# Linear attention, soft mixture of experts and FFN in one kernel: expert weights placed anew, slot denominators moved ahead, the FFN's first tile by quarters

## The chip, the core and the metric

The kernel runs on one core of a Trainium2 chip. Five engines work in parallel, each on its own instruction queue: TensorE (PE, matrix products; its weight loads are shown as PEld), VectorE (DVE), ScalarE (ACT), GpSimd (Pool) and SyncE (SP), which in this kernel issues all DMAs. They are tied together by semaphores only: an instruction waits until a counter has reached a value. PE writes its results to PSUM, eight banks of 128 x 512 fp32; DVE and ACT carry them to SBUF. The metric is the time of one execution on the device in microseconds; lower is better. It is given as the median of several runs.

## What is computed

Three stages, cut to the core:

```python
def attn(r, k, v, w, u):            # B, H, S, D = 4, 8, 768, 48
    for t in range(S):
        kv = einsum('bhd,bhe->bhde', k[t], v[t])
        y[t] = einsum('bhd,bhde->bhe', r[t], state + u * kv)
        state = w * state + kv

def moe(x, phi, w1, w2):            # x: 3072 x 384, 8 experts with 4 slots each, F = 1024
    logits = x @ phi                              # 3072 x 32
    d = exp(logits - logits.max(0)); d /= d.sum(0)      # over the tokens
    slot_in = d.T @ x                             # 32 x 384
    slot_out[e] = relu(slot_in[e] @ w1[e]) @ w2[e]
    c = exp(logits - logits.max(1)); c /= c.sum(1)      # over the slots
    return c @ slot_out

def ffn(x, w_in, w_out):            # 384 -> 2048 -> 384
    h = x @ w_in
    return where(h > 0, h, exp(min(h, 0)) - 1) @ w_out
```

## The kernel before

**Attention** runs over 24 units: 6 chunks of 128 tokens times 4 batches (`un = c * B + b`). For each unit SP loads r, k and v (192 KB each), Pool multiplies them by decay tables (L435 to L453), PE turns them and forms scores, outputs and states, and DVE and ACT carry results along. SP issues everything in one order, written out in `load_chunk`: with every unit also one piece of the first expert weight, `load_w1(un)` (L329, 24 pieces of 512 KB in all). A load of r and k for unit un + 4 waits for `bonus_ready` and `k_scaled`, a load of v for `y_done`.

**Expert stage.** After the last unit DVE forms the softmax over the tokens (`col_w`) and over the slots (`row_w`), PE sums the slots' inputs (L618, `x_sb` weighted by `col_w`, with one column of ones for the denominators), and DVE turns the sums into `slot_T` through `den_cols`, `slot_parts` and `den_inv`. `row_parts` holds `row_w` split in a rounded part and a rest, each twice; PE turns it to `c_T`. The experts work in two groups of four: `expert_in(g, n)` (L635), a ReLU on ACT and DVE, `expert_turn` and `expert_out` (L654), which waits at its first four products for `w2_loaded[e]`. The order on PE is in(0), in(1), out(0), first half of out(1), turn of group 0's result, second half of out(1), turn of group 1's. The second expert weights (`w2_sb`, 8 of 1536 KB, L366) are loaded into places that other tensors leave: 0 and 1 where r and k were, 2 to 4 over `x_sb` after the slot sums (`PE_SLOT_IN`), 5 to 7 over w1 after `h_done` 1 and 2. Behind them in SP's queue come `w_in` (3 of 1 MB, L384) and, after `so_done` 1, `w_out` (4 of 768 KB, L388).

**FFN.** Since x @ w_in is c @ (slot_out @ w_in), the kernel forms G = slot_out @ w_in (L704, a 32 x 2048 matrix, kept as four row groups of bank 3, one for each 512 columns), splits it into a rounded part and a rest (`G_parts`) and spreads each group over 128 rows by two matmuls with 0/1 matrices (`spread`, L718), so that `G_T` (128 x 2048) meets `c_T` in one product. `ffn_in(i, f)` (L712) then gives tile f (128 of the 2048 columns of h) of chunk i (512 tokens). Each tile passes exp (ACT L1109), relu(1 - exp) (ACT L1096), max(h, 0) minus that (DVE L973), rounding to `elu_hi` (DVE L986) and the rest `elu_lo` (DVE L965), and enters the output by 12 matmuls (L753 to L755): for each of four batches hi x w_out_hi, hi x w_out_lo, lo x w_out_hi. There are 96 tiles, 16 for each of 6 chunks. `w_out_high(f)` on ACT (L1084) rounds w_out's rows, and Pool forms the rest `w_out_lo` (L461), in the first chunk only. All orders are written out by hand; `RING = 4` banks hold h.

## Time and profile before

| | |
|---|---|
| runs | 411.21 us median of 3 (410.6 to 412.23) |
| profiled execution | 413.13 us, of which the span (first to last instruction) is 410.8 |
| granted TensorE clock, mean | 0.992 |
| PE busy | 388.4 us (95%) |
| DVE busy | 275.1 us (67%) |
| ACT busy | 221.2 us (54%) |
| Pool busy | 117.5 us (29%) |
| read from HBM | 45.86 MB |

The page of the profile gives each engine's busy time and, in 40 slices of the span (10.3 us each), its busy share in tenths, the clock that TensorE was granted (9 is 90% or more of full speed) and the share of the 16 DMA engines that was busy. Roughly: attention until 132 us, the softmaxes and experts until 175, G and the first tiles until 195, the FFN loop to the end. The trace gives every instruction with its start, its duration and what it waited for.

### The profile page before, as it was taken

To read this page: it belongs to the slowest core of one execution; us is meant where nothing else is said; L and a number is where in the kernel's file an instruction comes from. 1 tells how busy PE (TensorE), PEld (TensorE's weight loads), DVE (VectorE), ACT (ScalarE), POOL (GpSimd) and SP (SyncE) were. 2 spreads that over 40 slices of the span, in tenths; PEclk is the share of its full clock that TensorE was granted. 3 is DMA by queue.
4 is the path that set the end of the run, shared out by engine and by line. 5 is a ranking of instruction groups with operands and counts; after the bars stand their busy time and mean duration, and the time that the engine had idled before them with its cause. 6 is when DMAs were issued, how large, how long until landed. Compare 5 with 4: busy or idle time off the path is not lost.

```text
span 410.8 us, 9542 instructions
## 1 busy us (share of the span) xinstructions
PE 388.4 (95%) x3529; PEld 343.2 (84%) x3529; DVE 275.1 (67%) x517; ACT 221.2 (54%) x503; POOL 117.5 (29%) x131
## 2 busy tenths in 40 slices
PE   6699999999998798769999999999999999999997
PEld 6588888888885344238999999999999999999996
DVE  4687777777764920049997677676767767676771
ACT  1676767676763216057665545645554564546441
POOL 4997878787850000018530000000000000000000
PEclk9899999999999999899999999999999999999999
DMA  6999999999977499950002000200020020002002
GB/s 126 204 234 228 245 234 239 237 225 243 218 231 300 145 429 356 406 201 2 0 2 77 2 1 2 77 0 0 0 77 0 0 77 0 0 0 77 2 0 77
DMA packets 86530, 51.05 MB, mean 124 GB/s; under 512 B 76768, under 2 KB 82016, under 8 KB 85088
## 3 DMA queue, kind: packets, MB, share of 16 engines
q1 hardware_dynamic: 86496, 50.59, 42.9%
q8 instruction: 23, 0.38, 0.4%
q14 instruction: 11, 0.09, 0.1%
HBM read 45.86 MB, written 4.72 MB: 123 GB/s over the span
## 4 chain that ended last, share of the span: by engine, by line
PE 88%; DVE 4%; DMA 3%; POOL 1%; issue 1%; ACT 1%; SPq 0%; POOLq 0%; DVEq 0%
PE psum L753 16%; PE psum L754 16%; PE psum L755 16%; PE psum L504 6%; PE psum L535 6%; PE psum L712 5%; PE psum L543 3%; DMA w<-in_moe_w_dram 3%; PE psum L516 3%; PE psum L486 3%; PE psum L635 3%; PE psum L493 3%; PE psum L526 2%; PE psum L654 2%; PE psum L550 1%
## 5 line engine op out<-in xcount | busy, mean ns | idle before, releaser
L753 PE MATMUL psum<-w_out_hi,elu_hi 128*128 128x384 f32 x384 | 129.3, 337 | 1.1 <-DVE elu_lo L965 1.1
L754 PE MATMUL psum<-w_out_lo,elu_hi 128*128 128x384 f32 x384 | 129.0, 336 | 0.0
L755 PE MATMUL psum<-w_out_hi,elu_lo 128*128 128x384 f32 x384 | 128.3, 334 | 0.0
L1109 ACT ACTIVATE exp_h<-psum 128x512 f32<-128x512 f32 x96 | 57.6, 601 | 98.3 <-PE psum L712 98.3
L973 DVE SCALAR_TENSOR_TENSOR elu<-psum,neg_part 128x512 f32<-128x512 f32 x96 | 66.2, 690 | 54.5 <-ACT neg_part L1096 54.4
L753 PEld LDWEIGHTS psum<-w_out_hi,elu_hi 128*128 128x128 f32 x384 | 72.1, 188 | 3.7 <-DVE elu_lo L965 2.5
L754 PEld LDWEIGHTS psum<-w_out_lo,elu_hi 128*128 128x128 f32 x384 | 72.0, 188 | 3.3
L755 PEld LDWEIGHTS psum<-w_out_hi,elu_lo 128*128 128x128 f32 x384 | 72.1, 188 | 0.0
L965 DVE TENSOR_TENSOR elu_lo<-elu,elu_hi 128x512 fp32r<-128x512 f32 x96 | 66.3, 691 | 0.1
L1096 ACT ACTIVATE neg_part<-exp_h 128x512 f32<-128x512 f32 x96 | 59.9, 625 | 0.0
L1004 ACT ACTIVATE scores<-ident,bonus 128x128 f32<-128x128 f32 x192 | 58.7, 390 | 0.8 <-DVE bonus L804 0.7
L986 DVE CAST elu_hi<-elu 128x512 fp32r<-128x512 f32 x96 | 49.7, 517 | 0.1
L814 DVE COPY_PREDICATED scores<-mask,psum 128x512 f32<-128x512 uint32 x48 | 35.4, 740 | 14.1 <-ACT scores L1004 13.6
L461 POOL TENSOR_TENSOR w_out_lo<-w_out_raw,w_out_hi 128x384 fp32r<-128x384 f32 x16 | 20.2, 1277 | 73.5 <-ACT w_out_hi L1084 73.5
L712 PE MATMUL psum<-c_T,G_T 128*128 (+1 forms) x96 | 37.4, 393 | 1.0 <-DVE elu L973 1.0
L504 PE MATMUL psum<-r_pair,k_pair 64*128 64x128 f32 x384 | 28.8, 290 | 1.8 <-DVE k_pair L809 0.9
L504 PEld LDWEIGHTS psum<-r_pair,k_pair 64*128 64x128 f32 x384 | 24.3, 193 | 3.9 <-issue 1.8
L453 POOL TENSOR_TENSOR k_nat<-k_raw,k_table 128x384 f32<-128x384 f32 x23 | 23.1, 1004 | 12.2 <-PE psum L526 12.2
L535 PE MATMUL psum<-scores,v_sb 128*64 128x128 f32 x384 | 26.3, 279 | 0.0
L440 POOL TENSOR_TENSOR r_raw<-r_raw,u_row 128x384 f32<-128x384 f32 x24 | 24.5, 1019 | 6.1 <-DVE r_nat L796 4.3
L1009 ACT COPY y_T<-psum 128x512 f32<-128x512 f32 x24 | 14.1, 586 | 22.2 <-PE psum L535 22.2
L442 POOL TENSOR_TENSOR r_raw<-r_raw,k_raw 128x384 f32<-128x384 f32 x24 | 24.0, 1001 | 1.9
(126 smaller groups left out, 409.0 us busy)
## 6 DMA issues: line engine op xcount, KB each, us to landing
w_sb<-in_moe_w_dram SPq DMA_DIRECT2D x24, 512.0 KB, 4.9
w<-in_moe_w_dram SPq DMA_DIRECT2D x8, 1536.0 KB, 9.8
r_raw<-in_r_dram SPq DMA_DIRECT2D x24, 192.0 KB, 4.6
k_raw<-in_k_dram SPq DMA_DIRECT2D x24, 192.0 KB, 5.1
v_sb<-in_v_dram SPq DMA_DIRECT2D x24, 192.0 KB, 5.3
out_dram<-out_sb SPq DMA_DIRECT2D x24, 192.0 KB, 1.9
w_in_sb<-in_moe_w_in_dram SPq DMA_DIRECT2D x3, 1024.0 KB, 16.0
w_out_raw<-in_moe_w_out_dram SPq DMA_DIRECT2D x4, 768.0 KB, 14.2
```

Of the source, the lines that this page charges most:

```text
L504: m = pe.matmul(ps_A[two][:, a, :], k_pair[rows, i, a, :], r_pair[rows, i, a, :], start=True, stop=True)
L535: m = pe.matmul(ps_y[e0:e0 + HP, two, (a // 2) * P:(a // 2) * P + P], v_sb[:, b, h, :], scores[:, i, h, :], start=(first and a < 2), stop= ...
L712: pe.matmul(banks[4 + f % RING][:, :], G_T[:, f * P:(f + 1) * P], c_T[:, bass.ds(i * BANK, BANK)], start=True, stop=True).then_inc(ffn_don ...
L753: pe.matmul(acc, hi, w_out_hi[:, f, :], start=(f == 0), stop=False)
L754: pe.matmul(acc, hi, w_out_lo[:, f, :], start=False, stop=False)
L755: m = pe.matmul(acc, lo, w_out_hi[:, f, :], start=False, stop=(f == KF2 - 1))
L965: dve.tensor_tensor(elu_lo[:, f % RING, :], elu[:, f % 2, :], elu_hi[:, f % RING, :].bitcast(F32), ALU.subtract).then_inc(lo_done, 1)
L973: dve.scalar_tensor_tensor(out=elu[:, f % 2, :], in0=banks[4 + f % RING][:, :], scalar=0.0, in1=neg_part[:, f % 2, :], op0=ALU.max, op1=AL ...
L986: dve.tensor_copy(elu_hi[:, f % RING, :], elu[:, f % 2, :]).then_inc(hi_done, 1)
L1004: m = act.activation(scores[:, i, h, :], ident[:, :], ACT.Copy, scale=bonus[:, i, h:h + 1])
L1096: act.activation(neg_part[:, f % 2, :], exp_h[:, f % 2, :], ACT.Relu, bias=1.0, scale=-1.0).then_inc(neg_ready, 1)
L1109: act.activation(exp_h[:, f % 2, :], banks[4 + f % RING][:, :], ACT.Exp).then_inc(exp_done, 1)
```

## The change

Five things, none of which changes the arithmetic of a result except the order in which w1's rows are added.

1. w1 is loaded in 8 pieces of 1536 KB, one for each expert, at units 1, 4, ..., 22, instead of 24 of 512 KB. Partition p holds the rows 3p to 3p+2 of an expert, so the slots' inputs are turned with a stride of three columns.
2. The second weights get other places. Weight 2 lies behind weights 0 and 1 and is loaded when the last unit's y is done; weights 3 and 4 lie over the first two thirds of `x_sb` and are loaded when PE has read 8 and 16 of its 24 units (`x_used`); 5 and 6 after `h_done` 1, 7 after `h_done` 2. `row_parts` moves behind 3 and 4, `w_out_lo` to the place of 5 and 6.
3. On DVE the slot denominators and `slot_T` come ahead of the sums of the rows.
4. G's split is on DVE alone, first 128 columns, then 384. Only the first 512 columns are spread by PE, with 32 rows instead of 128. The other 1536 columns of `G_T` are copied from `G_parts` by twelve DMAs of 32 x 512 (64 KB) on SP's queue; PE waits for them (`G_moved`) before tiles 4, 8 and 12 of the first chunk.
5. The first tile passes by quarters of 128 tokens, with its own semaphores: product, exp, relu, max-subtract, rounding, rest, and its three matmuls for each batch as soon as that quarter is there. In tiles 1 and 2 of the first chunk PE takes the eight products of `elu_hi` before the four of `elu_lo`.

```diff
         cursor[0] = max(cursor[0], LATE_AT)
+        w2_sb += [place("w2_2", [P, KF1, DM], F32)]
...
-        w2_sb += [place(f"w2_{e}", [P, KF1, DM], F32) for e in range(2, 5)]
+        w2_sb += [place(f"w2_{e}", [P, KF1, DM], F32) for e in range(3, 5)]
+        assert cursor[0] <= X_AT + 2 * UNITS // 3 * XW * 4
+        row_parts = place("row_parts", [P, UNITS, 4, SLOTS], F32R)
...
-        w1_dram = w1.rearrange("e (c p) f -> p (e c) f", p=P)
+        w1_dram = w1.rearrange("e (p c) f -> e p c f", p=P)
...
                     un = c * B + b
-                    load_w1(un)
+                    if un % KD == 1:
+                        load_w1(un // KD)
...
-            sp.wait_ge(pe_step, PE_SLOT_IN)
-            for e in range(2, 5):
-                load_w2(e)
+            sp.wait_ge(y_done, UNITS)
+            load_w2(2)
+            sp.wait_ge(x_used, 1)
+            load_w2(3)
+            sp.wait_ge(x_used, 2)
+            load_w2(4)
             sp.wait_ge(h_done, 1)
             load_w2(5)
+            load_w2(6)
             sp.wait_ge(h_done, 2)
-            for e in range(6, E):
-                load_w2(e)
+            load_w2(7)
...
+            sp.wait_ge(G_parts_ready, 4)
+            for n in range(1, F2 // BANK):
+                for j in range(GROUPS):
+                    sp.dma_start(G_T[j * GW:(j + 1) * GW, n * BANK:(n + 1) * BANK].bitcast(F32),
+                                 G_parts[n * GW:(n + 1) * GW, j % 2, :].bitcast(F32)).then_inc(G_moved[n], 16)
...
+                if n in (1, 3):
+                    m.then_inc(x_used, 1)
...
-            spread_G(0)
-            spread_G(1)
-            spread_G(2)
+            spread_G(banks[0][:, 0:P], slice(0, P))
             pe.wait_ge(cT_ready, UNITS // 4)
             pe.wait_ge(G_first_ready, 1)
-            ffn_in(0, 0)
-            spread_G(3)
-            for f in range(1, RING):
-                ffn_in(0, f)
-            pe.wait_ge(G_ready, F2 // BANK - 1)
+            ffn_in_first(0)
+            ffn_in_first(1)
+            pe.wait_ge(G_parts_ready, 4)
+            spread_G(banks[1][:, 0:BANK - P], slice(P, BANK))
+            ffn_in_first(2)
+            ffn_in_first(3)
...
+            pe.wait_ge(w_out_ready, 1)
+            first_out_high(0)
+            pe.wait_ge(G_rest_ready, 1)
+            for b in range(1, B):
+                pe.wait_ge(elu_first, b + 1)
+                ffn_in(0, b)
+                first_out_high(b)
+                first_out_low(b - 1)
+            first_out_low(B - 1).then_inc(parts_used, 1)
...
-            act.wait_ge(G_done, 1)
-            act.copy(G_parts[:, 0, :], banks[3][:, :]).then_inc(G_parts_ready, 1)
             w_out_high(0)
+            w_out_high(1)
             act.wait_ge(G_spread, 1)
-            act.copy(G_T[:, 0:BANK], banks[0][:, :]).then_inc(G_first_ready, 1)
+            act.copy(G_T[:, 0:P], banks[0][:, 0:P]).then_inc(G_first_ready, 1)
+            for b in range(B):
+                quarter = slice(b * P, (b + 1) * P)
+                act.wait_ge(h_first, b + 1)
+                act.activation(exp_h[:, 0, quarter], banks[4 + b][:, 0:P], ACT.Exp).then_inc(exp_first, 1)
+                act.wait_ge(exp_first, b + 1)
+                act.activation(neg_part[:, 0, quarter], exp_h[:, 0, quarter], ACT.Relu, bias=1.0, scale=-1.0
+                               ).then_inc(neg_first, 1)
```

In SP's queue behind attention, before (w2_n is expert weight n; the number behind the last underscore counts buffers):

```order
L366 DMA w2_1_81<-in_moe_w2_dram 128x3072
L366 DMA w2_2_97<-in_moe_w2_dram 128x3072 [waits pe_step]
L366 DMA w2_3_98<-in_moe_w2_dram 128x3072
L366 DMA w2_4_99<-in_moe_w2_dram 128x3072
L366 DMA w2_5_101<-in_moe_w2_dram 128x3072 [waits h_done]
L366 DMA w2_6_106<-in_moe_w2_dram 128x3072 [waits h_done]
L366 DMA w2_7_107<-in_moe_w2_dram 128x3072
```

and in SP's queue of the changed kernel, to the end of the loads:

```order
L382 DMA w2_1_81<-in_moe_w2_dram 128x3072
L382 DMA w2_2_82<-in_moe_w2_dram 128x3072 [waits y_done]
L382 DMA w2_3_97<-in_moe_w2_dram 128x3072 [waits x_used]
L382 DMA w2_4_98<-in_moe_w2_dram 128x3072 [waits x_used]
L382 DMA w2_5_101<-in_moe_w2_dram 128x3072 [waits h_done]
L382 DMA w2_6_102<-in_moe_w2_dram 128x3072
L382 DMA w2_7_105<-in_moe_w2_dram 128x3072 [waits h_done]
L403 DMA w_in_sb_108<-in_moe2_w_in_dram 128x2048 x3
L407 DMA w_out_raw_109<-in_moe2_w_out_dram 128x4x384 [waits so_done]
L407 DMA w_out_raw_109<-in_moe2_w_out_dram 128x4x384 x3
L413 DMA G_T_104<-G_parts_106 32x512 [waits G_parts_ready]
L413 DMA G_T_104<-G_parts_106 32x512 x11
```

Weights 2 to 4 wait for three earlier events instead of one, weight 6 goes with 5, and twelve copies of G stand behind w_out.

On DVE after the clearing of `slot_T`, before:

```order
L905 TENSOR_REDUCE row_sum<-row_w 128x24 [waits act_step]
L907 TENSOR_SCALAR row_sum<-row_sum 128x24 [waits dve_step]
L909 RECIPROCAL row_sum<-row_sum 128x24 [waits dve_step]
L911 TENSOR_TENSOR row_w<-row_w,row_sum 128x768 [waits dve_step]
L915 COPY den_cols<-psum 128x128 [waits pe_step]
L916 COPY slot_parts<-psum 128x384
L918 TENSOR_SCALAR den_inv<-psum 128x32 [waits pe_step]
L921 RECIPROCAL den_inv<-den_inv 128x32 [waits dve_step]
L924 TENSOR_TENSOR slot_T<-psum,den_inv 128x24x4 [waits pe_step,dve_step]
L930 CAST row_hi<-row_w 128x768 [waits dve_step]
```

and on DVE in the changed kernel:

```order
L975 COPY den_cols<-psum 128x128 [waits pe_step]
L976 COPY slot_parts<-psum 128x384
L978 TENSOR_SCALAR den_inv<-psum 128x32 [waits pe_step]
L981 RECIPROCAL den_inv<-den_inv 128x32 [waits dve_step]
L984 TENSOR_TENSOR slot_T<-psum,den_inv 128x24x4 [waits pe_step,dve_step]
L990 TENSOR_REDUCE row_sum<-row_w 128x24 [waits act_step]
L992 TENSOR_SCALAR row_sum<-row_sum 128x24 [waits dve_step]
L994 RECIPROCAL row_sum<-row_sum 128x24 [waits dve_step]
L996 TENSOR_TENSOR row_w<-row_w,row_sum 128x768 [waits dve_step]
L999 CAST row_hi<-row_w 128x768 [waits dve_step]
```

The four row steps have moved behind `slot_T`, on which PE waits.

On PE after G's sum, before:

```order
L718 MATMUL psum<-G_parts,spread 128x512 [waits G_parts_ready,spread_ready]
L718 MATMUL psum<-G_parts,spread 128x512 x5
L712 MATMUL psum<-c_T,G_T 128x512 [waits G_first_ready,cT_ready]
L718 MATMUL psum<-G_parts,spread 128x512 x2
L712 MATMUL psum<-c_T,G_T 128x512 x3
L712 MATMUL psum<-c_T,G_T 128x512 [waits elu_done,G_ready]
L753 MATMUL psum<-w_out_hi,elu_hi 128x384 [waits w_out_ready,lo_done]
```

and on PE in the changed kernel:

```order
L751 MATMUL psum<-G_parts,spread 128x128
L745 MATMUL psum<-c_T,G_T 128x128 [waits G_first_ready,cT_ready]
L745 MATMUL psum<-c_T,G_T 128x128
L751 MATMUL psum<-G_parts,spread 128x384 [waits G_parts_ready]
L751 MATMUL psum<-G_parts,spread 128x384
L745 MATMUL psum<-c_T,G_T 128x128 x2
L770 MATMUL psum<-w_out_hi,elu_hi 128x384 [waits hi_first,w_out_ready]
L770 MATMUL psum<-w_out_lo,elu_hi 128x384
L740 MATMUL psum<-c_T,G_T 128x512 [waits elu_first,G_rest_ready]
L770 MATMUL psum<-w_out_hi,elu_hi 128x384 [waits hi_first]
...
L775 MATMUL psum<-w_out_hi,elu_lo 128x384 [waits lo_first] x2
L740 MATMUL psum<-c_T,G_T 128x512 [waits G_moved1]
```

The first output matmul stands behind 128-column steps only, and ffn_in(0, 4) waits for copied pieces of G.

## Rows read from the trace of the kernel before

**Rows 1.** Page, the span in 40 slices: granted clock and DMA share, in tenths

```profile
PEclk9899999999999999899999999999999999999999
DMA  6999999999977499950002000200020020002002
```

**Rows 2.** Timeline and tile view, attention: start us, us, engine, line; us to landing

```profile
92.66 0.38 SPq L322 DMA_DIRECT2D r_raw<-in_r_dram  x1
...
DMA to landing us min/median/max: 3.1/4.6/5.0
...
101.03 1.02 POOL L435 TENSOR_TENSOR r_nat<-r_raw,r_table 128x384 f32<-128x384 f32 x1
```

**Rows 3.** Timeline, 134 to 145 us: PE, DVE, ACT

```profile
134.60 4.10 PE L618 MATMUL psum<-x_sb,col_w 128*32 128x386 f32 x48 [1.44 <-ACT col_w L1044]
...
137.12 0.95 DVE L905 TENSOR_REDUCE row_sum<-row_w 128x24 f32<-128x768 f32 x1
...
139.54 0.28 DVE L915 COPY den_cols<-psum 128x128 f32<-128x128 f32 x1
...
140.32 0.30 ACT L1049 CAST ident_r<-ident 128x128 fp32r<-128x128 f32 x1 [3.23 <-PE psum L623]
...
142.94 1.75 DVE L934 TENSOR_TENSOR row_parts<-row_w,row_hi 128x1536 fp32r<-128x1536 f32 x1
```

**Rows 4.** Timeline of expert_out on PE; then windows (busy, clock, DMA share, GB/s)

```profile
156.67 6.39 PE L654 MATMUL psum<-w,hidden_T 128*32 128x384 f32 x70
...
165.94 4.30 PE L654 MATMUL psum<-w,hidden_T 128*32 128x384 f32 x26 [2.89 <-DMA w<-in_moe_w_dram]
...
170.76 2.79 PE L654 MATMUL psum<-w,hidden_T 128*32 128x384 f32 x32
...
168.00:169.00 1.00, 1.00 (x9) 0.36 (x2) 0.00 (x0) 0.00 (x0) 0.00 (x0) 0.50 1.01 426
```

**Rows 5.** DMA issues on SP, w2 and w_out: first and last start; us to landing

```profile
w<-in_moe_w_dram SPq DMA_DIRECT2D x1, 1536.0 KB, 6.1
...
L366 SPq DMA_DIRECT2D w<-in_moe_w_dram x2: 432/432/432, 139.1 to 139.6; - x2
...
DMA to landing us min/median/max: 9.5/11.8/14.2
...
L366 SPq DMA_DIRECT2D w<-in_moe_w_dram x1: 328/328/328, 147.1 to 147.1; - x1
...
DMA to landing us min/median/max: 10.2/10.2/10.2
...
L366 SPq DMA_DIRECT2D w<-in_moe_w_dram x2: 327/380/433, 153.5 to 153.9; - x2
...
DMA to landing us min/median/max: 8.7/10.3/12.0
...
L388 SPq DMA_DIRECT2D w_out_raw<-in_moe_w_out_dram x4: 378/1373/6626, 162.1 to 169.7; - x4
...
w_out_raw<-in_moe_w_out_dram SPq DMA_DIRECT2D x1, 768.0 KB, 11.9
```

**Rows 6.** Timeline and chain, 177 to 196 us; last, phi's issues (us to landing)

```profile
177.91 0.59 ACT L1087 CAST G_parts<-psum 128x512 fp32r<-128x512 f32 x1 [3.81 <-PE psum L704]
...
184.57 0.44 PE L753 MATMUL psum<-w_out_hi,elu_hi 128*128 128x384 f32 x1 [0.62 <-DVE elu_lo L965]
...
187.61 0.44 PE L753 MATMUL psum<-w_out_hi,elu_hi 128*128 128x384 f32 x1 [0.45 <-DVE elu_lo L965]
...
190.06 1.23 DVE L986 CAST elu_hi<-elu 128x512 fp32r<-128x512 f32 x1
...
185.99 7.59 POOL L461 TENSOR_TENSOR w_out_lo<-w_out_raw,w_out_hi 128x384 fp32r<-128x384 f32 x6 [0.41 <-ACT w_out_hi L1084]
...
195.38 0.18 PE psum L753
...
phi_sb<-in_moe_phi_dram SPq DMA_DIRECT2D x4, 12.0 KB, 2.3
```

More of the change, by code:

```diff
@@ new lines, in _, with first_out_high, first_out_low @@
+            ffn_in_first(2)
+            ffn_in_first(3)
+            def first_out_high(b):
+                pe.wait_ge(hi_first, b + 1)
+                for n, w_part in enumerate((w_out_hi, w_out_lo)):
+                    pe.matmul(banks[b][:, 0:DM], elu_hi[:, 0, b * P:(b + 1) * P], w_part[:, 0, :],
+                              start=(n == 0), stop=False)
+            def first_out_low(b):
+                pe.wait_ge(lo_first, b + 1)
+                return pe.matmul(banks[b][:, 0:DM], elu_lo[:, 0, b * P:(b + 1) * P], w_out_hi[:, 0, :],
+                                 start=False, stop=False)
@@ L743, in ffn_group @@
                         ffn_in(i + 1, f + RING - KF2)
-                    pe.wait_ge(lo_done, q + 1)
+                    if first and f == 0:
+                        continue
+                    if first and f <= 2:
+                        pe.wait_ge(hi_done, q)
+                        pe.wait_ge(w_out_ready, f + 1)
+                        for b in range(B):
+                            for w_part in (w_out_hi, w_out_lo):
+                                pe.matmul(banks[b][:, 0:DM], elu_hi[:, f % RING, b * P:(b + 1) * P], w_part[:, f, :],
+                                          start=False, stop=False)
+                        pe.wait_ge(lo_done, q)
+                        for b in range(B):
+                            m = pe.matmul(banks[b][:, 0:DM], elu_lo[:, f % RING, b * P:(b + 1) * P], w_out_hi[:, f, :],
+                                          start=False, stop=False)
+                        m.then_inc(parts_used, 1)
+                        continue
+                    pe.wait_ge(lo_done, q)
                     if first:
@@ new lines, in first_lo @@
+            def first_lo(b):
+                dve.wait_ge(hi_first, b + 1)
+                return dve.tensor_tensor(elu_lo[:, 0, quarter(b)], elu[:, 0, quarter(b)],
+                                         elu_hi[:, 0, quarter(b)].bitcast(F32), ALU.subtract).then_inc(lo_first, 1)
+            first_elu(0)
+            first_hi(0)
+            dve.wait_ge(G_spread, 2)
+            dve.tensor_copy(G_T[:, P:BANK], banks[1][:, 0:BANK - P]).then_inc(G_rest_ready, 1)
+            for b in range(1, B):
+                first_elu(b)
+                first_lo(b - 1)
+                first_hi(b)
@@ L975, in ffn_group @@
                                              ).then_inc(elu_done, 1)
[L976 removed]
+                    if not (first and f <= 2):
                         elu_lo_of(i, (f - 1) % KF2, q - 1)
[L978 removed]
+                    dve.wait_ge(elu_done, q)
                     if f >= RING:
```

150 lines of the change are left out of this document (90 added, 60 removed).

## Prediction, written before the changed kernel ran

> **What bounds the kernel now.** I read the slices first [rows 1]: TensorE's granted clock is at the upper level (2.4 GHz) nearly everywhere, with one dip in the seventeenth slice, and the DMA share is at its ceiling up to about 123 us and again from 139 to 180 us, with a hole between. Then the chain of waits: it is TensorE for 88% of the span, but between 138 and 188 us it passes through VectorE's softmax rows, through one DMA of 12.0 us (expert weight 7), and through the hand-overs ACT to DVE to ACT at the head of the FFN. From 195.4 us on it is TensorE alone. So every microsecond by which that point comes earlier is a microsecond of the kernel, and nothing after it matters. The FFN loop itself is not changed. I therefore work out when expert weight 7 is there, when G is there, and when the fifth FFN tile (f = 4) starts.
>
> **Attention stage.** The 24 pieces of w1 (512 KB) become 8 (1536 KB) at units 1, 4, ..., 22. The bytes are the same; what has been issued ahead of a load of r differs by one old piece at most, early or late, which at 430 GB/s is 1.2 us. The load of r for unit 20 is issued at 92.66 and lands 4.6 us later (median, 5.0 at most), and Pool first reads it at 101.03 [rows 2]: 3.4 to 3.8 us to spare, and no engine in this stage waits for a DMA. Cost: nothing, hidden by those 3.4 us. Without that cover it costs what a load comes late, eight times; that is the rival on the slow side. Below zero it could bring little, since nothing there waits for a transfer; I allow 0.3.
>
> **Slot denominators first.** VectorE does row_sum (0.95, with two short steps after it) and the row_w product before den_cols; PE's slot sums (L618) are ready at 138.7, but den_cols starts at 139.54 [rows 3]. Moved behind slot_T, the row steps free the path: gain 139.54 - 138.72 = **0.8**. The row steps take 2.5 us, so row_parts ends near 142.94 + 1.75 + 2.5 - 0.8 - 0.2 = 146.2 instead of 144.7. Who waits for that: the ReLU of `hidden` on the same queue, which can't start before expert_in(0) is done at 147.1 - 0.8 = 146.3, and the weights' turn on PE at 153. Both hide it. Were the cover gone it would be 0.1 or so.
>
> **Expert weights.** Group 1's first half is 32 records of L654, and the second half shows what 32 cost: 2.79 us. Group 0 ends at 162.0, so the half should end at 164.7; its last 26 records start at 165.94 and take 4.30, until 170.25 [rows 4]. Lost: **5.5** us. 26 records at 2.79/32 are 2.27, so 2.0 of the 5.5 is the clock: PE was idle from about 163 to 165.9 and the granted clock was 0.50 (1.2 GHz) in 168 to 169 [rows 4]. The other 3.5 is the wait.
> Does weight 7 come in time now? Landings before [rows 5]: weight 2 issued 138.75 into an empty queue, 6.1 later; 3 and 4 at 148.6 and 153.8; 5 at 157.3; 6 at 162.2; 7 at 165.9. In a full queue they are 3.5 to 5.2 apart, mean 4.1. After: weight 2 is issued behind 1 as soon as the last unit's y is done, some 6 us ahead of the rest; weight 3 at the first x_used (8 of the 24 units of L618 [rows 3], 134.6 + 4.1 x 8/24 = 136.0), weight 4 at 137.4. They fill the hole and land by about 146.3. 5 and 6 go at expert_in(0)'s end, 146.3, into a queue just empty: 152.4 and 156.5. 7 follows at 160.6 (159.4 to 162.6 by the two ends of the interval). PE first wants it 0.2 us into group 1, which is now 162.0 - 0.8 + 0.2 = 161.4. So the wait becomes 0 to 1.2; I take 0.2, nearest to the mean interval. What is late next is w_in: 1 MB each, 2/3 of 4.1 apart, the last at 168.8, wanted at 170; it hides. Gain 5.5 - 0.2 = **5.3**. G's sum then ends at 177.9 - 0.8 - 5.3 = 171.8.
>
> The Trainium skill, "DMA: Bandwidth & Descriptors" (Latency and other measured facts), says that two of the sixteen DMA engines are usually slower in traces. The landings agree so far as they can: the mean rate shows weights 2 to 5 moved by 155.5, while weight 5 is only reported at 157.3. By the mean rate alone weight 7 would be there near 158 and the 0.2 would be 0.
>
> **Head of the FFN, with T = end of G's sum.** Before, T = 177.9: G_parts starts at T+0.0 and the first output matmul at T+6.7 [rows 6]. After, the same steps are 128 columns wide: 0.30 on ACT, 0.28 on VectorE from PSUM [rows 3], about 0.3 for one matmul. In a row: two on VectorE (T+0.65), spread with PE's start (T+1.2), G_T on ACT (1.6), product (2.0), exp and relu (2.65), max-subtract and rounding (3.2): first output matmul at **T+3.35**. That is not the gain. VectorE then has one 384-wide copy and ten 128-wide steps in a row, about 0.27 each: until T+6.5. Only then comes tile 1, full width, and there VectorE is already the limit before: PE starts tile 1 at 187.61, right behind elu_lo, and the period is 2.58 because the rounding step takes 1.23 instead of 0.43 while Pool runs w_out_lo [rows 6]. Pool is just as busy after. I lay it out: tile 1's rounding ends T+7.65 and its low part T+8.35; tile 2's T+10.1 and 11.3; tile 3's low part, 2.6 on, T+14.1. PE: tile 0 done T+7.0 (before T+8.9), tile 1 T+9.85, tile 2 T+12.3, then it waits for tile 3's low part until T+14.15, and starts tile 4 at T+16.5 to 16.7. Before that was 195.38, T+17.5. Gain 17.5 - 16.6 = **0.9**. Ends: 0, if the many narrow steps cost 0.1 more each; and 1.9, the lead at the end of tile 0 kept whole.
>
> The Trainium skill, "SBUF — State Buffer" (Who interferes with whom), says that VectorE's copies in a two-port mode, and its operations with two inputs in SBUF, exclude GpSimd for the whole instruction. The 1.23 agrees. By that rule the narrow steps of tile 0 run free, since ACT makes w_out_hi(2) only after them; it gives the same sum.
>
> **G by DMA.** Three wide VectorE copies (1.93 in all) and six of eight spread matmuls go; twelve DMAs of 64 KB come, behind G_parts_ready 4 at T+1.9 on SP's queue. Behind them on SP are only the stores, 40 us later. PE waits for the first four before ffn_in(0, 4), wanted at T+7.0, harmful from T+7.25 = 179.0. No such transfer is in the trace; bounds: the four small phi loads take 2.3 us to land [rows 6], and w_out's four pieces are in the same queues ahead. Those landed last at 169.7 + 11.9 = 181.6 [rows 5], 15.7 behind weight 7, with the queue full all the way; after, 160.6 + 15.7 = 176.3. So the four pieces land between T+1.9 + 4 x 0.4 + 2.3 = 177.6 and, if they start only behind w_out, 176.3 + 2.3 = 178.6. Cost 0, with 0.4 to 1.4 us of cover; that is the thinnest cover of the change. w_out's first piece (landed 175.5 before) comes at 170.2, ahead of T, and its two roundings on ACT are off the path.
>
> By the skill's "DMA: Bandwidth & Descriptors" (Anatomy of one DMA) a DMA costs a fixed 2.0 us or so plus its bytes; four pieces by that page are an estimate of 2.6 us, at 177.9.
>
> **Sum.** 0.8 + 5.3 + 0.9 = 7.0. The profiled execution took 413.13 with a span of 410.8; it becomes 406.1. The median of the runs is 411.21, 1.9 below the profiled one, so the forecast is 411.21 - 7.0 = **404.2**.
>
> **Rivals.** (a) Forecast as above, 403.1 to 405.4: chance 0.56. (b) Expert weight 7 is late still: w2 intervals of 5 us and a slower start out of the empty queue, 1.5 to 4 us of wait, with 2.0 for the clock if PE is idle 3 us again. For it: intervals of 4.9 and 5.2 exist. Against: three weights leave 9 to 2 us earlier. Typical 404.2 + 2.5 = 406.7, at worst 410.2: 0.15. (c) G's pieces wait behind w_out, or cost more than the phi loads: 1 to 3 us of PE waiting at tile 1, 406.2: 0.13. (d) The clock falls in the sparse stretch T to T+4, where PE has some 1.5 us of work; before, with 3 to 4 us in the first 6, it stayed at 1.00. At half clock tiles 0 and 1 cost 2 more: 406.2: 0.03. (e) The head gains its full lead, since PE works on high parts while VectorE catches up: 411.21 - 0.8 - 5.5 - 1.9 = 403.0: 0.08. (f) Slower: bursts of w1 in attention. A burst puts 1 MB more ahead of r (2.4 us), and if a queue that is full cannot make this up in the two units without one, loads land over 3.6 us late. From 3.6 + 9.1/8 = 4.7 us late on, eight bursts eat the 7.0 and 2.1 more and the kernel is over 0.5% slower; at 5.0 us late they cost 11.2, 415.4: 0.03. (g) The change doesn't do what it says, no wait goes because slots 5 to 7 still follow h_done: gains 0.8 + 0.9, 409.5: 0.02.
>
> **Numbers.** The range 401.9 to 407.3 takes (a), (c), (d), (e) and most of (b), and 0.8 for the scatter of the runs shown. About 0.5% (2.1 us) is what a measurement of this kernel tells from no change: faster than 409.15 are (a), (c), (d), (e) and nearly all of (b): 0.92. Within: the rest of (b), (g), and half-way cases of (f): 0.05. Slower: 0.03.
>
> **What would show it.** den_cols starts at 138.7; the wait of L654 for DMA under 1 us and PEclk without its dip; G's first rounding near 172; the first output matmul 3.3 us later; the first full-width rounding on VectorE at T+7; PE's wait before ffn_in(0, 4) at zero; the fifth tile at T+16.6. Wrong would make it: Pool waiting for r or k in attention, a dip of the clock past T, or PE waiting on G_T's DMAs.

## Result and the profile after

| | before | changed |
|---|---|---|
| median of 6 runs each, same chip | 411.61 us | 407.33 us (405.83 to 408.89) |
| ratio, 95% interval | | 0.9896 (0.987 to 0.9923) |
| profiled execution, span | 413.13, 410.8 us | 407.67, 405.5 us |
| mean granted clock in it | 0.992 | 0.996 |
| PE busy | 388.4 us | 384.7 us |

The changed kernel is faster by 4.3 us (3.2 to 5.4 by the interval), not by 7.0, and its 407.33 lies just outside the range (to 407.3). A second measurement of it (a0 below) gives a ratio of 0.9888, or 4.6 us. The two profiled executions differ by more, 5.3 us of span. Two of the later runs of the kernel before took 959 and 1308 us, against 410 to 415 for the others, and are left out below.

The page of the changed kernel, granted clock and DMA share in 40 slices, against [rows 1]:

```profile
PEclk8999999999999999999999999999999999999999
DMA  6989899899987879970002000200100020002002
```

The dip in the seventeenth slice is gone. Of the hole in the DMA row (7, 4 in slices 13 and 14) 7, 8 is left, and slice 15 has fallen from 9 to 7: weights 2 to 4 are moved early, and the queue then runs empty until weights 5 and 6 are issued. In attention three of the slices 2 to 11 now read 8, where all ten read 9.

Timeline of TensorE in the changed kernel (start us, us, engine, line, operation, [idle before <- releaser]), to be read against [rows 3, 4, 6]:

```profile
135.66 4.10 PE L644 MATMUL psum<-x_sb,col_w 128*32 128x386 f32 x48 [1.44 <-ACT col_w L1146]
...
140.62 1.24 PE L654 MATMUL psum<-fold,slot_parts 128*128 128x32 f32 x6
142.37 7.93 PE L663 MATMUL psum<-w_sb,slot_T 128*32 128x512 f32 x72 [0.51 <-DVE slot_T L984]
...
157.34 8.74 PE L682 MATMUL psum<-w,hidden_T 128*32 128x384 f32 x96
...
166.49 2.79 PE L682 MATMUL psum<-w,hidden_T 128*32 128x384 f32 x32
...
174.39 0.40 PE L751 MATMUL psum<-G_parts,spread 32*128 32x128 f32 x2 [0.83 <-DVE G_parts L1030]
...
176.93 0.41 PE L770 MATMUL psum<-w_out_hi,elu_hi 128*128 128x384 f32 x1 [0.36 <-DVE elu_hi L1044]
...
187.44 0.44 PE L823 MATMUL psum<-w_out_hi,elu_hi 128*128 128x384 f32 x1 [1.35 <-DVE elu_lo L1063]
...
190.02 0.44 PE L823 MATMUL psum<-w_out_hi,elu_hi 128*128 128x384 f32 x1
```

And three rows of VectorE: the slot denominators, G's first rounding, a full-width rounding while Pool is busy:

```profile
139.81 0.29 DVE L975 COPY den_cols<-psum 128x128 f32<-128x128 f32 x1 [1.61 <-PE psum L644]
...
173.63 0.29 DVE L1028 CAST G_parts<-psum 128x128 fp32r<-128x128 f32 x1 [2.91 <-PE psum L732]
...
187.31 1.24 DVE L1088 CAST elu_hi<-elu 128x512 fp32r<-128x512 f32 x1
```

Milestones, before minus after (positive is gained), from these rows and those ahead of the prediction:

| milestone | before | after | gained | forecast |
|---|---|---|---|---|
| slot sums start | 134.60 | 135.66 | -1.06 | 0 |
| expert_out starts | 156.67 | 157.34 | -0.67 | 0.8 |
| second half of expert_out, group 1 | 170.76 | 166.49 | 4.27 | 6.1 |
| G's first rounding (T) | 177.91 | 173.63 | 4.28 | 6.1 |
| fifth FFN tile | 195.38 | 190.02 | 5.36 | 7.0 |
| end of the span | 410.8 | 405.5 | 5.3 | 7.0 |

The -0.67 at expert_out is -1.06 from attention, +0.77 from the denominators and -0.38 from the strided turn (1.24 us in the row of L654). The loop behind the fifth tile gave nothing and took nothing. The profile has two losses ahead of the experts, which the prediction did not have, and one within them. The medians differ by 4.3, another microsecond less.

**Where the 1.06 arose.** ACT's copies of y, first and last unit, in the changed kernel:

```profile
20.75 0.59 ACT L1111 COPY y_T<-psum 128x512 f32<-128x512 f32 x1 [1.92 <-PE psum L561]
...
130.84 0.59 ACT L1111 COPY y_T<-psum 128x512 f32<-128x512 f32 x1 [2.38 <-PE psum L561]
```

Before, they stood at 21.72 and 129.79: the stretch is 110.09 us instead of 108.07. What Pool waited for, and the issues on SP around two bursts (start, us in which SP was held by the issue):

```profile
POOL r_nat L461 <- DMA k_raw<-in_k_dram: 5.1, 6, 1.9
```

```profile
20.75 5.05 SPq L341 DMA_DIRECT2D v_sb<-in_v_dram  x1
...
34.15 4.19 SPq L338 DMA_DIRECT2D k_raw<-in_k_dram  x1
38.38 3.75 SPq L341 DMA_DIRECT2D v_sb<-in_v_dram  x1
...
51.41 4.56 SPq L341 DMA_DIRECT2D v_sb<-in_v_dram  x1
```

The 24 issues of v on SP (duration of one, min/median/max in ns), before and in the changed kernel:

```profile
L326 SPq DMA_DIRECT2D v_sb<-in_v_dram x24: 367/2006/3337, 5.1 to 113.5; - x24
```

```profile
L341 SPq DMA_DIRECT2D v_sb<-in_v_dram x24: 367/1106/5047, 5.6 to 114.6; - x24
```

In the profile of before, Pool waited for no DMA in this stage. Issues of v held SP there too, 2.0 us in the median and 3.3 at most; the 0.38 of [rows 2] is one issue of r. With the large pieces the median issue is shorter and the longest ones, behind a burst, take 4 to 5 us. The slowest load of r lands after 7.7 us instead of 5.0, the slowest of k after 9.5 instead of 6.5. Pool waits six times, 1.9 us at most. The waits alone don't measure the cost: with 24 pieces Pool waits as well in some executions, 7.7 us in all in e1's profile, with a stretch of 108.4, and 7.2 in k1's.

### The profile page after: what moved, and what is told of

Same layout as the page of the kernel before. It is cut to its first block, busy times and chain, and to the rows that moved or that the text cites. A ratio compares the mean times of both kernels' runs of the same rounds, so it can differ in the third digit from the quotient of the medians.

```text
span 405.5 us, 9559 instructions
## 1 busy us (share of the span) xinstructions
PE 384.7 (95%) x3528; PEld 341.6 (84%) x3528; DVE 275.8 (68%) x527; ACT 219.3 (54%) x502; POOL 114.7 (28%) x131
## 4 chain that ended last, share of the span: by engine, by line
PE 87%; DVE 5%; issue 3%; POOL 3%; ACT 2%; DMA 0%; SPq 0%; DVEq 0%; POOLq 0%; ACTq 0%
PE psum L823 16%; PE psum L824 16%; PE psum L825 16%; PE psum L530 6%; PE psum L740 5%; PE psum L561 5%; PE psum L569 3%; PE psum L542 3%; PE psum L682 3%; PE psum L663 3%; PE psum L512 2%; PE psum L519 2%; PE psum L552 2%; PE psum L576 2%; PE psum L644 1%
## 5 line engine op out<-in xcount | busy, mean ns | idle before, releaser
L823 PE MATMUL psum<-w_out_hi,elu_hi 128*128 128x384 f32 x372 | 124.8, 336 | 1.3 <-DVE elu_lo L1063 1.3
L824 PE MATMUL psum<-w_out_lo,elu_hi 128*128 128x384 f32 x372 | 125.0, 336 | 0.0
L825 PE MATMUL psum<-w_out_hi,elu_lo 128*128 128x384 f32 x372 | 124.3, 334 | 0.0
L824 PEld LDWEIGHTS psum<-w_out_lo,elu_hi 128*128 128x128 f32 x372 | 69.8, 188 | 3.6
L823 PEld LDWEIGHTS psum<-w_out_hi,elu_hi 128*128 128x128 f32 x372 | 69.8, 188 | 2.1 <-DVE elu_lo L1063 2.1
L1063 DVE TENSOR_TENSOR elu_lo<-elu,elu_hi 128x512 fp32r<-128x512 f32 x95 | 69.9, 735 | 0.1
L825 PEld LDWEIGHTS psum<-w_out_hi,elu_lo 128*128 128x128 f32 x372 | 69.9, 188 | 0.0
L1088 DVE CAST elu_hi<-elu 128x512 fp32r<-128x512 f32 x95 | 41.5, 437 | 0.1
L740 PE MATMUL psum<-c_T,G_T 128*128 (+1 forms) x95 | 37.1, 392 | 0.1
L487 POOL TENSOR_TENSOR w_out_lo<-w_out_raw,w_out_hi 128x384 fp32r<-128x384 f32 x16 | 17.4, 1107 | 69.5 <-ACT w_out_hi L1183 69.5
L461 POOL TENSOR_TENSOR r_nat<-r_raw,r_table 128x384 f32<-128x384 f32 x23 | 23.2, 1010 | 5.1 <-DMA k_raw<-in_k_dram 5.1
```

Of the source, the lines that this page charges most:

```text
L740: pe.matmul(banks[4 + f % RING][:, :], G_T[:, f * P:(f + 1) * P], c_T[:, bass.ds(i * BANK, BANK)], start=True, stop=True).then_inc(ffn_don ...
L823: pe.matmul(acc, hi, w_out_hi[:, f, :], start=(f == 0), stop=False)
L824: pe.matmul(acc, hi, w_out_lo[:, f, :], start=False, stop=False)
L825: m = pe.matmul(acc, lo, w_out_hi[:, f, :], start=False, stop=(f == KF2 - 1))
L1063: dve.tensor_tensor(elu_lo[:, f % RING, :], elu[:, f % 2, :], elu_hi[:, f % RING, :].bitcast(F32), ALU.subtract).then_inc(lo_done, 1)
L1088: dve.tensor_copy(elu_hi[:, f % RING, :], elu[:, f % 2, :]).then_inc(hi_done, 1)
```

## Experiments

All ran with profiles beside runs of the kernel before on the same chip. Three sets: before was 413.11 in the first, 411.52 in the second, 412.96 in the third (medians). Only ratios are compared across sets. All kernels compute the whole result. "Stretch" is the time from the first to the last copy of y.

**e4: only w1's eight pieces and the stride, in the kernel before**

```diff
-        w1_dram = w1.rearrange("e (c p) f -> p (e c) f", p=P)
+        w1_dram = w1.rearrange("e (p c) f -> e p c f", p=P)
...
-                    load_w1(un)
+                    if un % KD == 1:
+                        load_w1(un // KD)
...
-                m = pe.matmul(banks[3][:, c * SLOTS:(c + 1) * SLOTS], slot_parts[:, c * P:(c + 1) * P], fold[:, :],
+                m = pe.matmul(banks[3][:, c * SLOTS:(c + 1) * SLOTS], slot_parts[:, c::KD], fold[:, :],
```

> The kernel before with only w1's part of the change: 8 pieces at units 1, 4, ..., 22, new row order, strided slot inputs. Theory 'bursts': 2.4 us slower than before, 414.0, with Pool waiting for r and k. Theory 'start': 0.4 us slower, 412.0.

Measured: 413.11 us, ratio 0.9994 (0.9968 to 1.002). Its profile, Pool's waits and the last copy of y:

```profile
POOL r_nat L436 <- DMA k_raw<-in_k_dram: 11.4, 7, 2.5
```

```profile
132.05 0.58 ACT L1010 COPY y_T<-psum 128x512 f32<-128x512 f32 x1 [2.38 <-PE psum L536]
```

This profile has the longest stretch of all, 111.1 us, and attention ends 2.3 us late. Yet the median does not move, where 0.4 or 2.4 us of loss were expected: by the upper end of the interval the bursts and the stride together cost 0.8 us at most in the median, well under what this profile shows.

**e1: the changed kernel with w1 loaded as before; e3: with eight pieces, but the old rows; a0: the changed kernel again**

e1 takes back both edits of e4. e3 takes back the stride alone (rows of w1 as before, still 1536 KB a piece):

```diff
-        w1_dram = w1.rearrange("e (p c) f -> e p c f", p=P)
+        w1_dram = w1.rearrange("e (c p) f -> p (e c) f", p=P)
...
-                sp.dma_start(w1_sb[:, e * KD:(e + 1) * KD, :], w1_dram[e]).then_inc(w1_loaded, 16)
+                sp.dma_start(w1_sb[:, e * KD:(e + 1) * KD, :], w1_dram[:, e * KD:(e + 1) * KD, :]).then_inc(w1_loaded, 16)
```

> The changed kernel once more, unchanged, as the reference for the others of this call. Theory 'bursts' (w1 in eight pieces of 1536 KB makes Pool wait for r and k in attention, about 2 us in all): y of the last unit is copied near 130.8 us if the start of the kernel is as early as in the profiled run (first y at 20.8), and later if the start is as before (first y at 21.7), so the stretch from the first to the last y copy is again about 110.1 us against 108.1 before. Theory 'start' (the 2 us are chance of one profiled run): that stretch falls back to 108 to 109. Time 407.3 either way.

> The changed kernel with w1 as before: 24 pieces of 512 KB, old row order, slot inputs turned without a stride. Everything else is the change. Theory 'bursts': the stretch from first to last y copy is 108.1 again, no wait of Pool for a DMA, and the six transposing matmuls take 0.87 instead of 1.25 us; together 2.0 + 0.4 = 2.4 us less, 404.9. Theory 'start': only the 0.4 us of the stride, 406.9.

> The changed kernel with w1 still in 8 pieces but in the old row order, so that the slot inputs are turned without a stride, and each piece consists of runs of 4 KB instead of 12 KB. Theory 'stride': 0.4 us less than the changed kernel, in the six matmuls that turn the slots' inputs (0.87 us for six instead of 1.25): 406.9. Theory 'run length' (the long runs of 12 KB are what delays r and k): the 2.0 us of attention come back too, 404.9.

Measured: a0 407.7 (ratio 0.9888, 0.9847 to 0.9929), e1 407.75 (0.9886, 0.9839 to 0.9934), e3 408.85 (0.9903, 0.9868 to 0.9937). By the times none differs from another. e1 reached neither of its forecasts (404.9 or 406.9), e3 neither of its (406.9 or 404.9), and a0's stretch of 109.0 us lies between the two theories. So on the median, giving back both edits of w1 gained nothing. The profile of e1 shows one loss that the others do not have there. Windows of e1 over the head of the FFN (busy time of each engine, clock, DMA share, GB/s):

```profile
174.00:181.00 7.00, 6.95 (x22) 6.01 (x23) 5.47 (x18) 5.79 (x15) 0.78 (x2) 0.54 0.62 176
```

In e1 the clock stood at its lower level (1.2 GHz) for seven microseconds of the head, and from the start of the spread to the product of tile 8 it took 15.77 us instead of the 15.24 of the changed kernel. a0's profile had no dip at all. That is one execution each; over their six runs e1 and a0 have nearly the same mean clock (0.9905 and 0.9912), so the clock does not account for e1's missing gain on the median, and that stays open. The cost of the stride inside the kernel, however, is settled: the six products that turn the slots' inputs, weight loads and matmuls, first in the changed kernel, then in e3:

```profile
L654 PEld LDWEIGHTS psum<-fold,slot_parts x6: 251/262/263, 140.6 to 141.5; 128*128 128x128 f32 x6
L654 PE MATMUL psum<-fold,slot_parts x6: 337/340/362, 140.6 to 141.5; 128*128 128x32 f32 x6
```

```profile
L654 PEld LDWEIGHTS psum<-fold,slot_parts x6: 186/192/192, 142.6 to 143.1; 128*128 128x128 f32 x6
L654 PE MATMUL psum<-fold,slot_parts x6: 276/276/297, 142.6 to 143.1; 128*128 128x32 f32 x6
```

The group takes 1.24 us with the stride and 0.85 without, in every kernel run here: **0.38** us on the path. e3's attention stretch is 109.92 us although its rows lie as before: the layout of the pieces is not needed for a long stretch, their size is enough.

**h1: the kernel before with the new places and loads of the second weights and the denominators first.** w1, the FFN and G as before.

```diff
-            sp.wait_ge(pe_step, PE_SLOT_IN)
-            for e in range(2, 5):
-                load_w2(e)
+            sp.wait_ge(y_done, UNITS)
+            load_w2(2)
+            sp.wait_ge(x_used, 1)
+            load_w2(3)
...
-         D_ROWSUM, D_ROWEPS, D_ROWINV, D_ROWW, D_DENCOLS, D_SLOT_PARTS, D_DENEPS, D_DENINV, D_SLOT_T,
+         D_DENCOLS, D_SLOT_PARTS, D_DENEPS, D_DENINV, D_SLOT_T, D_ROWSUM, D_ROWEPS, D_ROWINV, D_ROWW,
```

> The kernel before with only the second weights' places and loads and the slot denominators first; w1 and the head of the FFN as before. Theory 'expert wait' (most of the gain is the wait for weight 7 and the slow clock behind it): G's spread starts 5.8 us earlier on the stage clock, that is 43.5 to 44 us after the last y copy instead of 49.6, and the head from there to the product of tile 8 takes 15.6 as before; 411.2 to 413.1 minus 5.8: about 406.5. Theory 'head' (the quarters bring the larger part): less than 4 us of gain, over 408.

Measured: 408.23, ratio 0.9916 (0.9887 to 0.9945). Timeline of TensorE:

```profile
134.60 4.10 PE L627 MATMUL psum<-x_sb,col_w 128*32 128x386 f32 x48 [1.44 <-ACT col_w L1054]
...
140.94 7.93 PE L646 MATMUL psum<-w_sb,slot_T 128*32 128x512 f32 x72 [0.51 <-DVE slot_T L925]
...
155.91 8.60 PE L665 MATMUL psum<-w,hidden_T 128*32 128x384 f32 x96
...
173.52 1.63 PE L729 MATMUL psum<-G_parts,spread 128*128 128x512 f32 x6 [1.52 <-DVE G_parts L966]
```

The slot sums start at 134.60 as in [rows 3], and the first expert product at 140.94 instead of 141.71: the denominators give **0.77**, as forecast. The spread starts at 173.52 instead of 179.37, a gain of 5.85 up to T where the terms say 6.1. The 96 products take 8.60 us, 0.65 above full pace. So between these two profiles the two terms are right. On the median h1 gains only 3.3 us (2.3 to 4.7), and its 408.23 is what the other theory had said. This is the cleanest sign of what failed, for h1 has neither the bursts nor the stride nor the new head. h1's profile has no dip of the clock and is the fastest of its eight executions (407.36 to 409.66), while the profile of before (413.13) was slower than all six runs of the result above. Of h1's eight runs seven have a mean clock under 0.995, of the 16 of before in this set seven: the new loads did not bring a higher clock.

**e5: the changed kernel with all of G spread by TensorE, no DMAs**

```diff
-            sp.wait_ge(G_parts_ready, 4)
-            for n in range(1, F2 // BANK):
-                for j in range(GROUPS):
-                    sp.dma_start(G_T[j * GW:(j + 1) * GW, n * BANK:(n + 1) * BANK].bitcast(F32),
...
             ffn_in_first(3)
+            spread_G(banks[0][:, :], slice(0, BANK), 3)
+            spread_G(banks[2][:, :], slice(0, BANK), 1)
+            spread_G(banks[3][:, :], slice(0, BANK), 2)
```

> The changed kernel with G's other 1536 columns spread by six matmuls and copied by three 512-wide VectorE copies (0.64 us each), as before, instead of twelve DMAs. Theory 'VectorE bounds the head': the 1.9 us of copies fall in the row of narrow steps, tile 4 starts about 1.9 us later, and from spread's start to the product of tile 8 it takes 17.1 instead of 15.2. Theory 'DMA is the thin cover': the 0.4 us that PE waited for the first copied pieces goes, and the copies hide: 14.9.

Measured: 409.37, ratio 0.995 (0.9919 to 0.998). From the start of the spread to the product of tile 8 it takes 17.47 us, against 15.24. PE spends 1.6 us on six more products, and then waits again for VectorE, which has the three wide copies back in its row:

```profile
176.71 1.61 PE L746 MATMUL psum<-G_parts,spread 128*128 128x512 f32 x6
...
183.74 0.45 PE L802 MATMUL psum<-w_out_hi,elu_hi 128*128 128x384 f32 x1 [0.78 <-DVE elu_hi L1089]
```

That is what the first theory had said (17.1). G by DMA is worth 2.2 us in the head; with this order of spreads on TensorE the quarters lose to the head of before (15.61).

**e6 and e7: the same with the clock kept up.** Both put 11 small products of ones (some 3.2 us of TensorE) into its idle places: six before the slot sums, three before the spread, two behind it. e7 is the changed kernel with these; e6 has w1 as in e1 too. e6 was run a second time.

```diff
+            keep_up(6)
             pe.wait_ge(x_ready, UNITS)
...
+            keep_up(3)
             pe.wait_ge(spread_ready, 3)
```

> The changed kernel with w1 as before, and with eleven products of ones on PE in its idle stretches: six before the slots' sums, three before G's spread, two before the first quarter's product; they write a bank that nothing reads. Theory 'clock' (a part of the runs is up to 2 us longer because the granted clock falls to the lower level behind those sparse stretches, as it did in the run with w1 as before at 174 to 181 us): no dip after 25 us, mean clock 0.99 or more, less scatter, median 405.5 or below. Theory 'no clock': mean clock and median as in the run without them, 407.7.

> The changed kernel, w1 in eight pieces, with the same eleven products of ones. Against the run with w1 as before and the same products, with the clock taken out of the comparison, theory 'bursts' says 2 us slower (1.6 in attention by the stretch from first to last y copy, 0.4 by the strided slot inputs), about 407.0 against 405.3. Theory 'start' says 0.4 us.

> The fastest version again on this chip: the changed kernel with w1 as before and eleven products of ones. If its lead is real and not the luck of four runs: 405.4, with a scatter under 1.5 us, 1.5% under the kernel before and 0.5% under the changed kernel's 407.3 to 407.7.

Measured: e6 405.39, ratio 0.985 (0.9801 to 0.9899), again 406.15, ratio 0.9836 (0.9805 to 0.9867); e7 407.03, ratio 0.9884 (0.9827 to 0.9941). In e6's first profile:

```profile
155.94 7.95 PE L687 MATMUL psum<-w,hidden_T 128*32 128x384 f32 x96
```

Here weight 7 is not waited for at all (7.95 is 96 products at full pace). e6 is 1.6 us below e7 in one set, as the theory of the bursts had said (2 us), but e7's profile has its clock at 0.66 in 141 to 146 us and e6's second profile has the same dip. The mean clock over the four runs each is 0.9955 for e6 and 0.9930 for e7; times the span that is an estimate of 1.0 us. So most of the 1.6 can be the clock, and the rest for w1 is within the noise of four runs.

**k0, k1, k2: the kernel before again; it, with products of ones; h1 with them.** If the dip behind the wait for weight 7 costs 2.0, then keeping TensorE busy through that wait (14 products, 28 records of L475) should give it back. k1 has six more before the slot sums and six before the spread, k2 only these twelve.

```diff
             pe.wait_ge(hT_ready, 4)
+            keep_up(3, 14)
             expert_out(1, range(KF1 // 2))
```

> The kernel before, unchanged, for a second profile. Theory 'lottery' (the slow clock behind the wait for weight 7, which cost 2.0 us in the profiled run, is there in a part of the runs only): this profile may have it or not; if not, PE's last 26 records before the turn take 2.3 us instead of 4.3, G's spread starts 47.6 us after the last y copy instead of 49.6, and the span is near 409. Theory 'always': 4.3 us and 49.6 again.

> The kernel before with products of ones on PE: six before the slots' sums, fourteen (3.0 us) in the wait for weight 7, six before G's spread. Nothing else differs. Theory 'always': the slow clock behind the wait goes in every run, 2.0 us faster, 409.5 where before has 411.5. Theory 'lottery': it was there in about half of the runs, so the median gains 1 us or less, while the clock column is near 0.996 in all runs and they scatter less.

> The kernel before with the second weights' places and the slot denominators first, and twelve products of ones (six before the slots' sums, six before G's spread). Against e6, which differs by the quarters, G by DMA and the narrow spread, with the clock out of the comparison. Theory 'head worth 0.8' (from G's end to the product of tile 9, 0.7 at spread's start plus 0.1 later): 406.2 against 405.4. Theory 'head worth its forecast lead of 1.9': 407.3.

Measured: k0 412.71, ratio 0.9989 (0.9963 to 1.0014); k1 412.33, ratio 0.9992 (0.9968 to 1.0017); k2 408.48, ratio 0.9897 (0.9858 to 0.9937). Windows and timeline of k1:

```profile
143.00:146.00 3.00, 3.00 (x20) 0.97 (x16) 2.60 (x2) 0.00 (x0) 0.00 (x0) 0.54 1.04 442
167.00:170.00 3.00, 3.00 (x37) 1.70 (x39) 0.00 (x0) 0.00 (x0) 0.00 (x0) 1.00 0.99 415
```

```profile
142.62 9.63 PE L641 MATMUL psum<-w_sb,slot_T 128*32 128x512 f32 x72 [0.51 <-DVE slot_T L932]
...
164.56 3.39 PE L475 MATMUL psum<-ones 128*128 128x128 f32 x28
167.88 2.79 PE L660 MATMUL psum<-w,hidden_T 128*32 128x384 f32 x32
```

The dip behind the wait is gone, as meant (32 products in 2.79, not 4.30 for 26 as in [rows 4]). But another stands in the first expert products, which take 9.63 instead of 7.93. Weight 7 hangs on them, since its issue waits for `h_done`. The issues of weights 6 and 7 in k1 and their landing:

```profile
L366 SPq DMA_DIRECT2D w<-in_moe_w_dram x2: 328/380/433, 156.1 to 156.5; - x2
...
DMA to landing us min/median/max: 7.5/9.2/10.8
```

Weight 7 lands at 167.3 instead of 165.9, and the products of ones run until 167.9. The first half of group 1 starts only then, and ends at 170.7 instead of 170.2 although it runs at full pace. The median is that of the kernel before. The clock's 2.0 was removed at its place and did not leave the kernel; the 0.6 us by which the products outlast the landing make the trial less than clean.

k0's profile has the dip again (26 products in 4.08), which is what 'always' had said. k2 was to take 406.2 or 407.3 against 405.4 for e6; it took 408.48 against e6's 406.15 on the same chip. The head is then worth 2.3 us on these medians, of which the mean clocks (0.9908 and 0.9932) make some 1.0 by the same estimate.

The dips of e7, k1 and e6's second profile all begin at 141 to 143 us, behind the slot denominators: in k1 PE is busy for 1.30 of the 3 us before. No products of ones stood there. In e3, e4 and e5 a dip begins at 134 to 137 us, where PE had been idle before the slot sums; none of the five profiles with products of ones at that place has a dip there. But e6's first profile has the same idle place at the denominators and no dip, so idleness alone does not decide it.

## The clock, over all runs

Every run lists its span and mean granted clock. By set, so that like is compared with like:

| set, kernel | runs | mean clock | runs at 0.995 or more | median span, us |
|---|---|---|---|---|
| 1, before | 18 | 0.9906 | 3 | 410.9 |
| 1, changed (a0) | 6 | 0.9912 | 2 | 405.4 |
| 1, e1 | 6 | 0.9905 | 1 | 405.55 |
| 1, e3 | 7 | 0.9916 | 2 | 406.5 |
| 1, e4 | 12 | 0.9902 | 4 | 410.85 |
| 2, before | 16 | 0.9926 | 9 | 409.25 |
| 2, h1 | 8 | 0.9888 | 1 | 406.0 |
| 2, e5 | 10 | 0.9930 | 4 | 407.6 |
| 2, e6 | 4 | 0.9955 | 4 | 403.4 |
| 2, e7 | 4 | 0.9930 | 2 | 404.75 |
| 3, before | 22 | 0.9903 | 7 | 410.75 |
| 3, k0 | 10 | 0.9906 | 3 | 410.5 |
| 3, k1 | 10 | 0.9927 | 3 | 410.15 |
| 3, k2 | 5 | 0.9908 | 1 | 406.3 |
| 3, e6 again | 6 | 0.9932 | 4 | 403.9 |

A difference in mean clock times the span is an estimate of what the clock is worth in time, where TensorE bounds the kernel. The changed kernel against before in set 1: 0.0006 x 408 = 0.2 us; with e1 and e3, which have the same new loads of the second weights, the 19 runs have 0.9911 against 0.9906, again 0.2, give or take 1.1 by the scatter of the runs. h1 against before in set 2: 1.5 us lost, give or take 2.3. So the change takes little or no clock out of a typical execution, where the forecast had 2.0. Only the kernels with products of ones are higher than before by more: e6 by 1.2 us in both sets, k1 by 1.0, which does not show in its time; by its profile its products and the later weight 7 use it up.

How much a run gains by a high clock is itself unsteady. Runs of before at 0.995 or more have a median span of 411.0, 408.7 and 409.4 in the three sets, those below 410.8, 410.8 and 411.1.

In profiles: both of the kernel before and that of e4, which leaves the experts alone, have the dip behind the wait for weight 7. Of ten profiles of kernels with the new loads, none has it there, but five have one of 4 to 7 us elsewhere between 134 and 181 us, costing 0.5 to 1.7 each; five have none. So the dip went from its place and came back at others.

## Why the prediction was wrong

**What held.** The mechanisms and their places: den_cols at 139.81, directly behind the slot sums (0.77 for 0.8); the idle 2.89 us before L654 in [rows 4] gone; the first output matmul at T+3.3 (forecast 3.35) and the fifth tile at T+16.4 (forecast 16.5 to 16.7, before 17.5), so the head gave 1.1 for 0.9; VectorE's rounding again at 1.24 us beside Pool, as in [rows 6]; w_in and row_parts hidden. The narrow VectorE steps follow each other in some 0.2 us, not 0.27, and tile 0 is done at T+6.7 instead of T+7.0.

**G by DMA.** Forecast: four pieces at T+5.8 to T+6.8, wanted at T+7.0. The issues, and what product L740 waited for:

```profile
175.33 7.58 SPq L413 DMA_DIRECT2D G_T<-G_parts  x12
```

```profile
DMA to landing us min/median/max: 2.0/2.3/3.1
```

```profile
  DMA G_T<-G_parts: 0.4, 1
```

Each issue takes 0.59 us of SP, not 0.4, and the loads are there at T+6.7; PE wanted them at T+6.4 and waited 0.4. It is off the path, since PE then waits for tile 3's elu_lo anyway (187.44, 1.35 us). The cover of this term was thinner than said, the cost was 0 as said. In e6 and e7 PE waits 1.2 and 0.9 us for these pieces, and the head takes 15.3 us all the same. By the Trainium skill, "DMA: Bandwidth & Descriptors" (Anatomy of one DMA), the estimate was 2.6 us for four pieces. The page's figure of about 2.0 us and the bytes stands there for DMAs that GpSimd issues, and these go out from SP; the landings of 2.0 to 3.1 us agree with it for each piece, and the issues in a row made the four together take longer.

**Step that failed, 1: 2.0 us of clock inside the 5.3.** It was read from one window of one execution [rows 4] and subtracted from a median of others. That execution lay 1.9 us above the median of the runs shown, a difference the prediction named and then did not use. By the mean clocks above, the change gains some 0.2 us of clock, not 2.0; missing: 1.8 us (an estimate). h1, which has only these loads and the denominators, gains 3.3 us on the median where this term and that of the denominators say 6.1. The wait for the weight itself was right in the main: 2.89 us of idleness before the products became 0.66.

**Step that failed, 2: "Cost: nothing, hidden by those 3.4 us" in attention.** The cover was read at one unit of one execution. In other executions of kernels with the same 24 pieces Pool does wait for k (k0 1.5 us, k1 7.2, e1 7.7 in all), so it was not there for every unit. The bytes ahead were counted, and how long an issue holds SP's queue was not. The mean stretch is 109.7 us in the six profiles with bursts and 108.4 in the eight without. The last copy of y comes **0.7** us later on average, though the two groups overlap (129.6 to 132.0 against 129.3 to 130.7), and 1.06 in the profile. This is rival (f)'s mechanism at a fraction of its size. The other 0.5 is an earlier first copy, and this goes with the place of a dip at the start: it comes at 20.8 or 20.9 us where the clock fell at 8 or 9 us (also in e6's second profile, with 24 pieces) and at 21.7 to 21.9 where it fell at 17. On the medians the loss is not seen: e4 against before shows none, and e1 against a0 shows none. That SP's hold is how the lateness arises is read from the rows above; no run here took it away with the pieces left large.

**Not in the sum at all: the stride**, 0.38 us in the profiles. The edit was named in the change and given no price.

**Weight 7.** The forecast had it at 160.6, wanted 161.4. Issues of the second weights in the changed kernel (durations, first and last start; then landing):

```profile
L382 SPq DMA_DIRECT2D w<-in_moe_w_dram x2: 328/380/433, 147.8 to 148.1; - x2
DMA to landing us min/median/max: 8.1/9.8/11.4
```

```profile
DMA to landing us min/median/max: 9.1/9.1/9.1
```

The first pair is weights 5 and 6, the last line weight 7, issued at 154.2. 5 and 6 were issued at 147.8 instead of 146.3, by the 1.06 and 0.38 above, and landed after 8.1 and 11.4 us where 6.1 and 10.2 were counted; 7 landed at 163.3. TensorE's weight load for it:

```profile
163.31 0.16 PEld L682 LDWEIGHTS psum<-w,hidden_T 128*32 128x32 f32 x8 [0.66 <-DMA w<-in_moe_w_dram]
```

The 96 products took 8.74 us instead of 7.95: 0.8 us lost, where 0.2 was taken from an interval of 0 to 1.2. In the six profiles of kernels with the new loads and no products of ones it is 0.4 to 0.8, 0.55 in the mean, so 0.4 more than forecast; with products of ones it is 0 in three and 0.9 in one. The mean interval of 4.1 in the prediction was also too short: from weight 3 at 148.6 to weight 7 at 165.9 it is 4.3. And the DMA row of [rows 1] reads 9 up to 113 us, not 123; nothing in the sum hangs on that.

**The sum again.** In the profiled pair, where the dip of before is whole: 7.0 - 1.06 - 0.38 - 0.6 (weight 7) + 0.2 (head) = 5.2; measured 5.3. On the medians, as an estimate: 7.0 - 1.8 (clock) - 0.4 (weight 7) + 0.2 (head) = 5.0; measured 4.3 and 4.6. What is left for the bursts and the stride is 0.4 to 0.7, less than the 1.1 of the profiles and more than the nothing of e4 and e1; the medians do not settle it. Rival (b) came about in part, with 0.8 us of wait instead of its 1.5 to 4; (d) only in e1, where seven microseconds at the lower clock cost 0.5 in the head. That the forecast missed its range by a hair is chance; that it promised half as much again as came is not.

What stays open: why the dips come at different places in executions of one kernel, what w1's edits cost on the median, and why e1 does not gain by leaving them out.

**The fastest version measured** is e6: the change without its edits of w1, with 11 products of ones. 405.4 and 406.15 us in two sets, ratios 0.985 and 0.9836. The intervals overlap that of the changed kernel (0.9847 to 0.9929 in a0), so its lead over it, some 0.4%, is likely and not proved.

## What to carry over

A gain read from one profiled execution is worth on the median only what recurs: compare the granted clock over many runs of both kernels before you count a dip as a gain, since removing one place of idleness may only move the dip. Read a cover at every unit and in more than one execution. Before you merge small prefetches to large ones, look at how long the largest issue holds the queue and not only at the bytes; single loads behind it came later here although the bytes were the same. And give every edit a price, also a mere change of stride.
